# The dense stage of a recurrent-attention and expert kernel: six groups of 512 rows in place of eight of 384

## The reference, cut to what matters

```python
def _moe_ref(x, modality_id, w_gate, modality_bias, w1, w2):      # x: 3072 x 384
    ...
    for e in range(E):                                            # 8 experts, F = 1024
        mask = e_idx == e
        h = np.maximum(x[mask] @ w1[e], 0.0)
        out[mask] = gate_w[mask, None] * (h @ w2[e])

def _moe2_ref(x, w_gate, w_val, w_out):        # 384 -> 1536 -> 384
    g = x @ w_gate
    silu = g * (1.0 / (1.0 + np.exp(-g)))
    val = x @ w_val
    return (silu * val @ w_out).astype(np.float32)
```

## Time and profile before

| | us |
|---|---|
| median of 3 runs | 985.26 |
| lowest and highest | 984.20, 986.14 |
| profiled execution, its own time | 984.72 |
| span of the profiled execution (first to last instruction) | 983.0 |
| start of the dense stage in the span | 516.0 |
| end of its last gate and value products | 970.0 |

### The profile page before, as it was taken

One profiled execution on the slowest core, in us unless ns is written; L12 is line 12 of the kernel. 1 busy time (PEld: TensorE's weight loads), 2 busy tenths in 40 slices (PEclk: granted clock), 3 DMA queues, 4 the chain that ended last, 5 costly groups with the idle time before them and its releaser, 6 DMA issues.

```text
span 983.0 us, 15493 instructions
## 1 busy us (share of the span) xinstructions
PE 922.0 (94%) x5986; PEld 880.3 (90%) x5986; DVE 560.0 (57%) x960; ACT 376.2 (38%) x538; POOL 185.4 (19%) x207
## 2 busy tenths in 40 slices
PE   2699999999959999999999999999999999999996
PEld 0577888888849999999999999999999999999995
DVE  6999787755555666666654544444454544445442
ACT  8998897846343444444441111111111111111111
POOL 7236253532753111100000010100101010010101
PEclk9899999999959999999999999999999999999999
DMA  5555432120368987766511010100001010000000
GB/s 176 140 184 162 85 98 67 33 59 3 129 215 279 327 245 239 239 193 190 172 48 51 1 49 1 49 1 25 25 2 47 1 49 1 25 25 1 25 1 24
DMA packets 94262, 90.57 MB, mean 92 GB/s; under 512 B 27599, under 2 KB 89311, under 8 KB 94180
## 3 DMA queue, kind: packets, MB, share of 16 engines
q1 hardware_dynamic: 83044, 62.92, 21.5%
q0 software_dynamic: 4288, 14.18, 4.2%
q10 hardware_dynamic: 6848, 12.39, 3.8%
HBM read 69.72 MB, written 19.72 MB: 91 GB/s over the span
## 4 chain that ended last, share of the span: by engine, by line
PE 86%; ACT 5%; DVE 2%; issue 2%; DMA 2%; POOL 1%; SPq 0%; POOLq 0%; ACTq 0%; DVEq 0%
PE psum L2083 30%; PE psum L2095 15%; PE psum L2034 10%; PE psum L2047 10%; PE psum L1786 4%; PE psum L1795 4%; PE psum L1831 2%; PE psum L1776 2%; PE psum L1812 2%; PE psum L1834 2%; PE psum L1765 1%; PE psum L1767 1%; ACT L1384 1%; PE psum L2004 1%; DMA group_work<-in_w 1%
## 5 line engine op out<-in xcount | busy, mean ns | idle before, releaser
L2083 PE MATMUL psum<-xT_parts,w_parts 128*128 128x384 f32 x1728 | 318.5, 337 | 1.5 <-DVE xT_parts L1357 1.5
L2083 PEld LDWEIGHTS psum<-xT_parts,w_parts 128*128 128x128 f32 x1728 | 303.9, 188 | 1.8 <-issue 1.8
L1366 DVE TENSOR_TENSOR group_work<-group_work,psum 128x384 f32<-128x384 f32 x96 | 53.3, 555 | 234.9 <-ACT group_work L1743 234.9
L1743 ACT ACTIVATE group_work<-psum 128x384 f32<-128x384 f32 x96 | 47.2, 492 | 364.1 <-PE psum L2083 359.6
L2095 PE MATMUL psum<-w_parts,act_parts 128*128 128x384 f32 x864 | 168.0, 338 | 1.6 <-DVE act_parts L1373 1.6
L2095 PEld LDWEIGHTS psum<-w_parts,act_parts 128*128 128x128 f32 x864 | 152.3, 188 | 4.3 <-DVE act_parts L1373 4.3
L639 POOL DMA_INDIRECT out<-group_work,sorted_id x24 | 23.4, 977 | 535.3 <-ACT group_work L1750 530.4
L2034 PE MATMUL psum<-xT_parts,expert_parts 128*128 128x400 f32 x576 | 118.3, 350 | 1.3 <-DVE expert_parts L1308 1.3
L2047 PE MATMUL psum<-act_parts,expert_parts 128*128 128x400 f32 x576 | 114.9, 343 | 0.0
L2034 PEld LDWEIGHTS psum<-xT_parts,expert_parts 128*128 128x128 f32 x576 | 104.9, 190 | 1.6 <-DVE expert_parts L1308 1.4
L2047 PEld LDWEIGHTS psum<-act_parts,expert_parts 128*128 128x128 f32 x576 | 104.9, 188 | 0.2
(11 more groups left out here) (201 smaller groups left out, 1055.2 us busy)
## 6 DMA issues: line engine op xcount, KB each, us to landing
group_work<-in_w SPq DMA_DIRECT2D x128, 192.0 KB, 3.4
yT_scratch<-group_work ACTq DMA_DIRECT2D x8, 600.0 KB, 6.0
arena<-in_q_rows SPq DMA_DIRECT2D x24, 192.0 KB, 3.6
arena<-in_k_rows SPq DMA_DIRECT2D x24, 192.0 KB, 3.9
arena<-in_v_rows SPq DMA_DIRECT2D x24, 192.0 KB, 3.7
x_scratch<-x_all SPq DMA_DIRECT2D x24, 192.0 KB, 1.9
group_work<-yT_scratch SPq DMA_DIRECT2D x8, 576.0 KB, 3.8
xs_scratch<-group_work POOLq DMA_DIRECT2D x7, 576.0 KB, 4.9
```

Source lines behind the costliest of these rows:

```text
L1366: link(nc.vector.tensor_tensor(sig[:, w % 2, :], sig[:, w % 2, :], psum[:, w % 2, 0:GW], ALU.mult))
L2083: last = nc.tensor.matmul(psum[:, b, 0:GW], wt[:, i, k, f * P:(f + 1) * P], x_p[:, j, g % 2, k, 0:GW], start=(k == n == 0), stop=(k == KC ...
```

## The change

The dense stage gets a tiling of its own: TD = 4 tiles, ND = 6 groups, WD = 512 rows. The gate and value products have 512 moving columns, which fill a PSUM bank, and the ACT and DVE instructions of a step have 512 elements in each partition. The output products keep their shape, four tiles for each step in banks 4 to 7. The activation parts have three buffers (`act_d`). At the end, `gv` of the last step stands ahead of `dn` of the last step but two, and the output products of the last two steps are done together, tile by tile, so that each tile is finished as early as possible for its copy and store. The first yT load waits also until seven groups' rows are transposed, as the buffers of the dense stage now lie over those of the expert stage in another way. The products of the expert stage are unchanged; their buffers are laid out anew, and the dense weights' raw buffers move behind them.

```diff
+    TD = 4
+    ND = NT // TD
+    WD = TD * P
...
+        w_raw = st_sb("expert_raw", [P, RAW, PIECE])
+        x_p_0 = st_sb("xT_parts_0", [P, 2, KC, GE], F32R)
+        xg_0 = st_sb("x_rows_0", [P, TG, DM])
+        x_sort = st_sb("x_rows_sorted", [P, TG, DM])
+        xg_1 = st_sb("x_rows_1", [P, TG, DM])
+        y_sb = st_sb("y_columns", [P, 2, KC, GE])
+        xg_last = st_sb("x_last_rows", [P, 2, GW])
+        we_p = st_sb("expert_parts", [P, SLOTS, 2, PIECE], F32R)
+        x_p_1 = st_sb("xT_parts_1", [P, 2, KC, GE], F32R)
+        act_p = st_sb("act_parts", [P, 2, 2, GE], F32R)
...
+        ph("gap_0", [P, RAW * PIECE])
+        xd_0 = ph("dense_xT_parts_0", [P, 2, KC, WD], F32R)
+        yT_in = ph("dense_yT", [P, KC, WD])
+        ph("gap_1", [P, 2 * KC * GE + 2 * TG * DM - 3 * KC * WD])
+        sig = ph("dense_act", [P, 2, WD])
+        ph("gap_2", [P, TG * DM - 2 * WD])
+        osb = ph("dense_out", [P, 2, TD, DM])
+        ph("gap_3", [P, 2 * KC * GE + 2 * GW - 2 * TD * DM])
+        xd_1 = ph("dense_xT_parts_1", [P, 2, KC, WD], F32R)
+        act_d = ph("dense_act_parts", [P, 2, 3, WD], F32R)
...
-            link(nc.gpsimd.tensor_scalar(begin[:, 0:MG], tab[0:1, 1, 0:MG], float(GW), 16.0, ALU.is_lt, ALU.mult))
+            link(nc.gpsimd.tensor_scalar(begin[:, 0:MG], tab[0:1, 1, 0:MG], float(WD), 16.0, ALU.is_lt, ALU.mult))
...
             sp.wait_ge(s_yst, needed)
-            sp.dma_start(yT_in, yT_dram[:, 0:GW].rearrange("(k p) n -> p k n", p=P)).then_inc(s_gl0, 16)
+            sp.wait_ge(s_xTp, KC * (NG - 1))
+            sp.dma_start(yT_in[:], yT_dram[:, 0:WD].rearrange("(k p) n -> p k n", p=P)).then_inc(s_gl0, 16)
...
-                    if w >= 2:
-                        down_done(dve, w - 2)
-                    high, low = act_p[:, 0, w % 2, 0:GW], act_p[:, 1, w % 2, 0:GW]
+                    if w >= 3:
+                        down_done(dve, w - 3)
+                    high, low = act_d[:, 0, w % 3], act_d[:, 1, w % 3]
...
-                            last = nc.tensor.matmul(psum[:, b, 0:GW], wt[:, i, k, f * P:(f + 1) * P],
-                                                    x_p[:, j, g % 2, k, 0:GW], start=(k == n == 0),
+                            last = nc.tensor.matmul(psum[:, b, :], wt[:, i, k, f * P:(f + 1) * P],
+                                                    xd[g % 2][:, j, k], start=(k == n == 0),
...
-            for w in range(NG * FFC + 1):
-                g, f = divmod(w, FFC)
-                if w < NG * FFC:
-                    gv(w)
-                if w >= 1:
-                    dn(w - 1)
+            end = ND * FFC - 1
+            for w in range(end):
+                gv(w)
+                if 1 <= w < end - 1:
+                    dn(w - 1)
+            gv(end)
+            dn(end - 2)
+            for i in range(TD):
+                dn_tile(end - 1, i)
+                dn_tile(end, i).then_inc(s_ot, 1)
```

More of the change, by code:

```diff
@@ L633, in _ @@
             nc.gpsimd.tensor_copy(tab[0:1, 3, 0:1], begin[:, 0:1]).then_inc(s_need, 1)
-            for g in range(NG):
-                for i in range(TG):
-                    t = g * TG + i
+            for g in range(ND):
+                for i in range(TD):
+                    t = g * TD + i
                     pool.wait_ge(s_ob, t + 1)
@@ L849, in _ @@
             sp.sem_inc(s_yall, 1)
-            for g in range(1, NG):
+            for g in range(1, ND):
                 load_group_yT(g)
             for i in range(2):
-                sp.wait_ge(s_out[i], 16 * TG * (NG // 2))
+                sp.wait_ge(s_out[i], 16 * TD * (ND // 2))
         @block.vector
@@ L1298, in x_evac @@
                         dve.wait_ge(s_h, FC * (t - 1))
[L1299 removed]
+                high, low = x_p[x_slot(t)][:, 0, k], x_p[x_slot(t)][:, 1, k]
                 if t > 0:
@@ L1728, in _ @@
                 act_e.wait_ge(s_xTp, k + 1)
-                nc.scalar.activation(x_p[:, 0, 0, k], psum[:, x_bank(0, k), 0:GE], ACT.Copy).then_inc(s_xh, 1)
+                nc.scalar.activation(x_p[0][:, 0, k], psum[:, x_bank(0, k), 0:GE], ACT.Copy).then_inc(s_xh, 1)
             for t in range(NG - 1):
@@ L1742, in _ @@
                         act_e.wait_ge(s_act, w - 1)
-                    nc.scalar.activation(sig[:, w % 2, :], psum[:, w % 2, 0:GW], ACT.Sigmoid).then_inc(s_sig, 1)
+                    nc.scalar.activation(sig[:, w % 2, :], psum[:, w % 2, :], ACT.Sigmoid).then_inc(s_sig, 1)
                 if g == 0:
@@ L1746, in _ @@
                 if g >= 2:
-                    act_e.wait_ge(s_out[g % 2], 16 * TG * (g // 2))
-                for i in range(TG):
-                    act_e.wait_ge(s_ot, g * TG + i + 1)
+                    act_e.wait_ge(s_out[g % 2], 16 * TD * (g // 2))
+                for i in range(TD):
+                    act_e.wait_ge(s_ot, g * TD + i + 1)
                     nc.scalar.activation(osb[:, g % 2, i, :], psum[:, 4 + i, 0:DM], ACT.Copy).then_inc(s_ob, 1)
@@ L2086, in gv, with dn_tile @@
                 last.then_inc(s_gv, 1)
-            def dn(w):
+            def dn_tile(w, i):
                 g, f = divmod(w, FFC)
                 pe.wait_ge(s_act, w + 1)
[L2091 to L2098, removed]
+                if f == 0 and g > 0:
+                    pe.wait_ge(s_ob, (g - 1) * TD + i + 1)
+                for n, (a, c) in enumerate(PRODUCTS):
+                    last = nc.tensor.matmul(psum[:, 4 + i, 0:DM], act_d[:, a, w % 3, i * P:(i + 1) * P],
+                                            w_o_p[:, c, f, :], start=(f == n == 0),
+                                            stop=(f == FFC - 1 and n == len(PRODUCTS) - 1))
+                return last
@@ L2099, in dn @@
+            def dn(w):
+                for i in range(TD):
+                    last = dn_tile(w, i)
+                    if w % FFC == FFC - 1:
                         last.then_inc(s_ot, 1)
-                    elif i == TG - 1:
+                    elif i == TD - 1:
                         last.then_inc(s_o, 1)
             pe.wait_ge(s_ws, DP)
-            for w in range(NG * FFC + 1):
-                g, f = divmod(w, FFC)
-                if w < NG * FFC:
-                    gv(w)
-                if w >= 1:
-                    dn(w - 1)
+            end = ND * FFC - 1
```

61 lines of the change are left out of this document (31 added, 30 removed).

## The result

The changed kernel took 980.9 us (median of 6 runs, 980.01 to 982.66) where the kernel before took 985.7 (6 runs, 984.2 to 987.25): ratio 0.9961, 95% interval 0.9945 to 0.9977. A second comparison, on another occasion, gave 980.08 against 984.5: 0.9955 (0.9939 to 0.9972). So the change takes 4 to 5 us off by the medians, about 0.4%. The forecast was 975.1 us and a gain of 10.2.

A forecast was written before the change was run, and what follows sets the result against it. TensorE was taken as the bound, busy 94% of the span, each dense product paid in full. Terms of -6.4, 0, -1.8, -0.7 and -1.3 us sum to -10.2, from 985.26 to 975.1 us; range 969 to 981.5.

The forecast's parts named there:

- term 1: Dense gate and value products: 1728 become 1296 wider ones, with a fixed extra of 15.5 ns each; -6.4 us.
- term 2: Dense output products: they stay 864 with 384 columns, so nothing changes.
- 3, changes of group: Changes between dense groups: seven waits of 0.25 us vanish, as the activation chain is hidden by 0.33 us; -1.8 us.
- 4, start: Start of the dense stage: TensorE no longer waits for the first activation chain; -0.7 us.
- term 5: Tail: last gate products end 3.16 us earlier, the span ends 14.8 us after them instead of 12.96; -1.3 us.
- T: In the tail, the moment the last gate products end, now ahead of 36 output products instead of 18.
- Rival B: Gate and value products: the extra grows with the columns, 232 to 234 ns each; 979.4 to 981.4 us; chance 0.17.
- Rival C: Gate and value products: longer products leave the weight load room, taking little above 213.3 ns; 958 us; chance 0.08.
- Rival D: Gate and value products: extra grows beyond proportion with full PSUM bank and 2 KB row; 989.6 us at 240 ns; chance 0.05.
- Rival E: Changes of dense group: the activation chain isn't hidden; 981.4 us at 1 us late each; chance 0.03.

The follow-up runs named there:

- widths: Changed kernel with 512, 448, 384, 320, 256 and 192 columns in the six groups' gate and value products; 18 take 4.19, 3.66, 3.17, 2.65, 2.14, 1.99 us.
- types: Changed kernel with gate and value products in bfloat16 in three groups, fewer rows or columns in two; bfloat16 18 take 3.90, 2.94, 1.98 us at 512, 384, 256 columns.
- plain_tail: Changed kernel with the old order at the end, no joint tiles, third activation buffer kept; 982.24 us, ratio to before 0.9974.
- joint_tail_only: Kernel before, groups of 384 rows, with only the third activation buffer and the last two steps' output products joint; 982.39 us, ratio 0.9979.

## Why the prediction was right in direction and wrong in size

| term | forecast | measured |
|---|---|---|
| 1, gate and value products | -6.4 | 72 x 4.19 = 301.7, -1.2 |
| 2, output products (the last 36 are in term 5) | 0 | 828 at 176.2, not 175.3: +0.8 |
| 3, changes of group | -1.8 | no wait, normal pieces: -1.8 |
| 4, start | -0.7 | no wait: -0.7 |
| 5, tail, with the 3.2 us moved behind T | -1.3 | 14.84 for 12.96, less 3.2: -1.3 |
| sum | -10.2 | -4.2 (span, from the same start: -4.4) |

**The step that failed** is the choice in term 1: "I take a fixed 15.5 ns". The extra of 15.3 ns at 384 columns isn't a price for each product. Two thirds of it go with the columns: 384 x (0.445 - 0.417) = 10.8 ns, and about 5 are fixed. `widths` shows that, and `types` shows that this part goes with the operands' type: in bfloat16 it is gone. So 432 fewer products save 432 x 5 = 2.1 us and not 6.4, and the bound that I named, 233.7 ns, was nearly the value (232.8). What misled me was to take 2.4 GHz as given for the column and to look at what is left over. The line through 384 and 400 columns that I had worked out (0.44 ns a column, 232.1 at 512) was right, and I put it aside because of a scatter of 1.0 ns. That it came so near is in part luck, as 1 ns at one of its two widths moves its value at 512 by 8 ns; but the same scatter spoke against a fixed extra just as much. Rival B, with 979.4 to 981.4 us, is what came, though I gave it 0.17; 980.9 us lies in the stated range only because that was drawn to take in B.

Of the 2.1 us the profile shows 1.2. In the kernel before, 18 gate and value products take 3.14 us in groups 1 and 3 and 3.17 in group 2, 174.4 and 176.1 ns each, in turn with the moving operand's two buffers. In the new buffers 384 columns take 176.1 (`widths`) and the output products 176.2. So the rest of term 1 and all of term 2 are a difference of about 1 ns a product, which the prediction kept in its range. That it comes from where the buffers lie is not shown.

**Rival C** asked for a product near 213.3 ns and didn't come; fewer weight columns took only 2.6 ns off. **Rival D** needed 236.7 ns; the line through 256 and 448 columns gives 231.4 at 512, so the whole bank and the 2 KB row cost 1.4 ns at most. **Rival E** didn't come: the chain at the change of group was ready at 599.76, 0.37 us before TensorE by the timeline and 0.54 by the chain, in which the forecast of 0.33 was worked out.

**Terms 3, 4 and 5** came as worked out, term 5 to 0.1 us, and with experiments behind it: the joint order alone gives 1.8 us in the kernel before and 2.1 in the changed one. The regrouping without it gives 2.3 (`plain_tail`), which is the terms again: -1.8 - 0.7 for waits that vanished, -1.2 + 0.8 for the products, and +0.8 for a fourth tile in the tail (14.84 for 12.96, less 6 more output products behind the last gate products) add up to -2.1. So the products, which held most of the forecast, give 0.4 us net.

## What to carry to other kernels

Before a matrix product is made longer to save its fixed price, find out how much of that price is fixed: one kernel with a different width in each group gives the line in one run. With F32R operands a product cost 5 ns + 0.445 ns a column from 512 down to 256 columns, so going from 384 to 512 saved little here, and what the larger group gave is fewer changes of group and a longer cover for the activation chain. At the end of such a kernel, move the last input products ahead of as many output products as buffers allow, and finish tile by tile: that gain can be worked out to a few tenths of a microsecond from the chain.

## What the runs showed of the hardware that was not expected

- Products with both operands F32R cost 0.445 ns a column at a granted clock of 1.00, with both bfloat16 0.417 (`widths`, `types`); at 512 columns 232.8 and 216.7 ns, side by side in one kernel.
- An F32R product of 192 columns with 128 weight columns took 110.6 ns, where the line through the wider ones gives 90.
- F32R products with 64 contraction rows were slower than with 128: 4.38 us for 18 in place of 4.19, and the 128-row products between them 2.30 in place of 2.11.
- Half or a quarter of the weight columns took about 2.6 ns off a product of 232.8, though the weight load itself went from 188 ns to 134 and 108.
- At the passage from the expert to the dense stage TensorE idles 1.5 to 2.0 us; in one profile of eleven, the one with 2.04, the granted clock fell to the lower level for most of the next 4 us and the stage took 1.6 us longer. In `widths`, too, TensorE waited 1.82 us (until 840.73) for the act chain at the change to 192 columns, where narrow steps no longer cover that chain, and the granted clock from 841 to 845 was 0.57. In `joint_tail_only` the same idle time of 1.82 us, ahead of the dense stage, left it at 1.00. So the length of the idle time alone doesn't decide it.
- The part of the kernel ahead of the dense stage differed by up to 2.8 us between profiled executions (513.66 to 516.46), more than what most of these edits change.
